# Attention group 15 on stacked split products, x_lo ahead of the query scaling on POOL, and two weight splits behind the token mixer's split on ScalarE

## The reference, cut to what is computed

```python
# 1. gated linear attention (mLSTM), B=2, H=8, S=768, head_dim 40, step by step over t:
m_new = max(f + m, i);  f_stab = exp(f + m - m_new);  i_stab = exp(i - m_new)
C = f_stab * C + i_stab * outer(v, k);   n = f_stab * n + i_stab * k
y[t] = sigmoid(o_gate) * (C @ q) / max(|n @ q|, 1)
# 2. mixer block on x = y as (B, S, 320): over tokens (768 -> 256 -> 768), then channels (320 -> 1536 -> 320)
h = relu(xT @ w_tok1) @ w_tok2;  u = x + hT;  x = u + relu(u @ w_ch1) @ w_ch2
# 3. x + real(FFT over channels of FFT over tokens); layer norm; channel MLP (320 -> 1280 -> 320)
```

## Time and profile before

| | us |
|---|---|
| median of 3 runs | 372.11 (371.92 to 373.74) |
| the profiled execution | 373.46 |
| its span, first to last instruction | 371.60 |
| PE busy | 362.3 (98%) |
| DVE / ACT / POOL busy | 190.5 / 155.5 / 129.3 |

### The profile page before, as it was taken

One profiled execution on the slowest core, in us unless ns is written; L12 is line 12 of the kernel. 1 busy time (PEld: TensorE's weight loads), 2 busy tenths in 40 slices (PEclk: granted clock), 3 DMA queues, 4 the chain that ended last, 5 costly groups with the idle time before them and its releaser, 6 DMA issues.

```text
span 371.6 us, 6184 instructions
## 1 busy us (share of the span) xinstructions
PE 362.3 (98%) x2371; PEld 350.9 (94%) x2371; DVE 190.5 (51%) x403; ACT 155.5 (42%) x325; POOL 129.3 (35%) x128
## 2 busy tenths in 40 slices
PE   8999998999999999999999999999999999999996
PEld 3788897899999999999999999999999999999996
DVE  7878753655343442154951486447934475331321
ACT  4678797789673232011441144505305202320310
POOL 6348886988987100010045200734414000000000
PEclk9999999999999999999999999999999999999999
DMA  7978999661535000003032100614050101001000
GB/s 161 246 171 231 235 298 274 186 197 55 146 88 146 19 0 2 18 30 116 1 108 71 56 0 3 228 54 160 2 167 29 35 3 53 2 15 40 0 19 35
DMA packets 18752, 34.36 MB, mean 92 GB/s; under 512 B 2636, under 2 KB 7892, under 8 KB 18724
## 3 DMA queue, kind: packets, MB, share of 16 engines
q1 hardware_dynamic: 17652, 32.40, 30.7%
q0 software_dynamic: 352, 1.31, 1.3%
q10 hardware_dynamic: 720, 0.27, 0.4%
HBM read 29.35 MB, written 4.62 MB: 91 GB/s over the span
## 4 chain that ended last, share of the span: by engine, by line
PE 83%; ACT 4%; DMA 2%; DVE 1%; issue 1%; SPq 0%; ACTq 0%; DVEq 0%
PE ps L712 31%; PE ps L689 25%; PE ps L692 4%; PE ps L691 4%; PE ps L647 3%; PE ps L571 3%; PE ps L814 3%; PE ps L795 2%; PE ps L665 2%; DMA og<-in_o 2%; PE ps L556 2%; PE ps L625 1%; PE ps L581 1%; PE ps L544 1%; PE ps L527 1%
## 5 line engine op out<-in xcount | busy, mean ns | idle before, releaser
L1009 ACT ACTIVATE h_hi<-ps 128x384 fp32r<-128x384 f32 x88 | 43.2, 491 | 116.3 <-PE ps L692 116.2
L1259 DVE SCALAR_TENSOR_TENSOR h_lo<-ps,h_hi 128x384 fp32r<-128x384 f32 x88 | 48.8, 555 | 55.0 <-ACT h_hi L1009 53.7
L1265 DVE TENSOR_TENSOR xt<-ps,xt 128x320 f32<-128x320 f32 x24 | 11.8, 491 | 65.5 <-PE ps L712 65.5
L712 PE MATMUL ps<-ch_hi,h_hi 128*128 128x320 f32 x144 | 45.1, 313 | 0.0
L712 PE MATMUL ps<-ch_hi,h_lo 128*128 128x320 f32 x144 | 44.5, 309 | 0.0
L712 PE MATMUL ps<-ch_lo,h_hi 128*128 128x320 f32 x144 | 44.5, 309 | 0.0
L712 PE MATMUL ps<-m_hi,h_hi 128*128 128x320 f32 x120 | 37.4, 312 | 0.0
L712 PE MATMUL ps<-m_hi,h_lo 128*128 128x320 f32 x120 | 37.1, 309 | 0.0
L712 PE MATMUL ps<-m_lo,h_hi 128*128 128x320 f32 x120 | 37.0, 309 | 0.0
L689 PE MATMUL ps<-uT_hi,ch_hi 128*128 128x384 f32 x96 | 32.5, 338 | 0.3 <-DVE xt L1428 0.3
L689 PE MATMUL ps<-uT_lo,ch_hi 128*128 128x384 f32 x96 | 32.1, 335 | 0.0
(11 more groups left out here) (172 smaller groups left out, 888.4 us busy)
## 6 DMA issues: line engine op xcount, KB each, us to landing
ch_raw<-in_ch SPq DMA_DIRECT2D x11, 384.0 KB, 6.9
vk<-in_vk SPq DMA_DIRECT2D x12, 328.0 KB, 4.5
raw<-in_kq SPq DMA_DIRECT2D x16, 240.0 KB, 3.6
m_raw<-in_m SPq DMA_DIRECT2D x11, 320.0 KB, 4.5
kq<-in_kq SPq DMA_DIRECT2D x16, 192.0 KB, 5.0
og<-in_o SPq DMA_DIRECT2D x12, 160.0 KB, 4.9
x_scratch<-xt SPq DMA_DIRECT2D x12, 160.0 KB, 2.3
out<-xt SPq DMA_DIRECT2D x12, 160.0 KB
```

The costliest lines, as they stand in the source:

```text
L712: mm = pe.matmul(bank, h[hx][:, f, i * P:(i + 1) * P], w[wx][:, f], start=(f == 0 and hx == 0 and wx == 0), stop=(f == FCH[k] - 1 and hx = ...
L1009: act.activation(h[0][:, f], h_bank(k, f), ACT.Relu).then_inc(hhi_done, 1)
L1259: dve.scalar_tensor_tensor(out=h[1][:, f], in0=h_bank(k, f), scalar=0.0, in1=f32(h[0][:, f]), op0=ALU.max, op1=ALU.subtract).then_inc(hlo_ ...
L1265: dve.tensor_tensor(xt[:, tile], o_bank(n), xt[:, tile], ALU.add).then_inc(o_done, 1)
```

## The change

`STACKED` goes from 16 to 15, so products(15) take four stacked matmuls, and group 15 gets a load, a rounding and a subtraction of its own. The host lays out one more group of `kq3`. The buffers move, since chunk 7's `kq` is still in use by group 14: the odd `kq3` buffers now lie over `kq` of even chunks, the even `raw3` buffers over both. `load_qk` still runs up to chunk 7.

```diff
+SPLIT_BEHIND = (12, 13)
+STACK_FIRST = {13: (15,)}
-STACKED = 16
+STACKED = 15
...
-    raw3 = [[at(f"raw3_{x}_0", o + 2048 * x, [P, 4 * CH]),
+    raw3 = [[at(f"raw3_{x}_0", o + 4096 + 2048 * x, [P, 4 * CH]),
...
-    kq3 = [[at(f"kq3_{x}_{n}", o + (8192, 4096)[n] + 2048 * x, [P, 4 * CH], F32R) for n in range(2)]
+    kq3 = [[at(f"kq3_{x}_{n}", o + (8192, 0)[n] + 2048 * x, [P, 4 * CH], F32R) for n in range(2)]
...
                 if n < STACKED + 2:
-                    sp.wait_ge(qk_done, STACKED - 2)
+                    sp.wait_ge(qk_done, (NG // 2, STACKED)[n - STACKED])
...
-                if cc + 1 < STACKED // 2:
+                if cc + 1 <= STACKED // 2:
                     load_qk(cc + 1)
...
-                act.wait_ge(qk_done, max(n - 1, STACKED))
+                act.wait_ge(qk_done, n - 1)
...
-                    if m < N_CH2:
+                    if m < N_CH2 and m not in SPLIT_BEHIND:
                         split_hi(m)
...
             attend(13)
+            stack_hi(15)
             attend(14)
             mixed_hi(0)
+            for m in SPLIT_BEHIND:
+                split_hi(m)
             attend(15)
...
+                if g == 1 and cc == NC:
+                    result_lo(cc - 1)
+                for m in STACK_FIRST.get(n, ()):
+                    pool.wait_ge(xlo_done, cc)
+                    stack_lo(m)
                 if g == 1 and cc >= NC and c < NC - 1:
                     scale_q(cc + 1)
...
-                if g == 1 and cc >= NC:
+                if g == 1 and cc > NC:
                     result_lo(cc - 1)
```

## The result

| | before | after |
|---|---|---|
| median (us) | 371.94 (20 executions, 371.45 to 373.74) | 374.82 (20 executions, 372.5 to 377.99) |
| profiled execution, its own time | 373.46 | 375.56 |
| its span | 371.6 | 373.8 |
| mean granted clock | 1.000 | 0.991 |

The ratio is 1.0066 [1.0054, 1.0079], which is 2.5 us of loss [2.0, 2.9]. The forecast was +1.0 us, 373.1, with a range to 374.4: the sign was right and the size was not. The median lies above the range; 371.94 times the ratio is 374.4, just at its end. The wide spread is new too. The executions differ in their mean clock: five of the 20 have 0.998 or more, with a median of 372.8; nine have 0.995, with a median of 374.7; six have 0.991, with a median of 375.5. By these medians, the lower the mean clock, the longer the time.

A forecast was written before the change was run, and what follows sets the result against it. PE was taken to bound the kernel: −1.61 − 0.46 − 0.42 (old waits, shorter products) + 2.99 (new waits ahead of mix_back) + 0.5 (wait at products(16)) = +1.0 us, so 373.1; range 371.2 to 374.4.

The forecast's parts named there:

- The bound: PE, busy 362.3 of 371.6 us; a shift of its work at 76 us should reach the end whole.
- x_lo first: On POOL, x_lo ahead of qs, there at about 58.1: PE's 1.61 us wait goes, mix_tokens(0, 5) starts at 61.0.
- Loads of group 15: In SP's queue ahead of eAb and og: 2.0 us more (bounds 1.3 to 2.9); raw(15) at 60.2, og at 62.5.
- stack_hi(15) ahead of attend(14): On ACT, waits for raw(15): W(14) 4 us later, at 61.3, so in_chunk(14) starts at 65.0, not 63.8.
- Two splits behind hp: On ACT, two ch_hi moved behind hp take 1.5 us off the 4.59 us from gate to hp_hi.
- mix_back(0): On PE: starts at 66.7 against 66.22, +0.5, with about 3.0 us of waits between 62 and 66.7.
- stack_lo(15) on POOL: 2.7 us more on POOL makes stack_lo(16) late, at 76.1; products(16) on PE wait 0.5 us, start at 76.2, +1.0.
- my signs of being wrong: Wrong if raw(15) lands before 59, if products(16) have no wait, or if ACT waits for raw(17).
- Raw(17), rival (c): Raw(17), issued behind stack_lo(15), delays ACT and products(16): shift 2.1 to 5.9 us, 374.2 and more; chance 0.19 with slow queue.

The follow-up runs named there:

- e5: The kernel before, unchanged, profiled once more: 372.32 us, ratio 1.0002.
- e2: The kernel before with only the two changes of order (x_lo first, two splits behind hp_hi), no group 15: 371.64 us, ratio 0.9992.
- e4: The kernel before plus two unused 240 KB loads where the changed kernel issues raw(15): 374.88 us, ratio 1.0070.
- e6: The kernel before plus the two unused loads of e4 and eight unread matmuls on PE ahead of mix_tokens(0, 5): 374.88 us, ratio 1.0084.
- e3: The changed kernel with stack_hi(15) behind W(14) and the mask on ACT instead of ahead of them: 374.08 us, ratio 1.0052.
- e10: The changed kernel with eight unread matmuls in PE's wait ahead of in_chunk(14), run again beside e9 on one chip: 373.12 us, ratio 1.0034.
- e1: The changed kernel with eight unread matmuls put into PE's wait ahead of in_chunk(14): 373.97 us, ratio 1.0039.
- e9: The changed kernel, unchanged, run again beside e10 on one chip: 374.5 us, ratio 1.0080.
- e11: e2 plus six mask copies on ACT ahead of attend(14), making W(14) late without added loads: 374.49 us, ratio 1.0096.
- e12: e11 plus eight unread matmuls in PE's wait ahead of in_chunk(14): 373.18 us, ratio 1.0036.
- e7: The changed kernel with weight loads 9 and 10 issued a chunk later, behind raw(15), eAb and og: 371.87 us, ratio 0.9994.

## Why the prediction was wrong in size

By its own steps:

- **The bound.** Right. PE's row decides, and a shift at products(16) reaches the end: +2.58 us there (77.82 against 75.24), +2.2 in the span, so 0.4 was made up behind it.
- **x_lo first.** Right in mechanism: it runs at 57.4 (forecast 58.1) and PE's wait is gone. Wrong in worth: 1.61 us was one execution's value, e5 has 0.94. The smaller gain was always there to be had; the order alone (e2) shows 0.3 us, which can't be told from none.
- **Loads of group 15.** Right in place, a little large in size. I took 2.0 us in bounds of 1.3 to 2.9. Where ACT waited for og itself it came at 60.90 (e4), 61.29 (e6) and 61.33 (e3), against 59.70 and 59.73 without the loads (e5, e2): 1.2 to 1.6 us. (Against the 60.54 of the first trace it would be half of that or less.) Raw(15) was down by 58.8 to 59.6 in the runs of this form, not 60.2. The Trainium skill (DMA: Bandwidth & Descriptors, Specifications) gives about 358 GB/s for a core, from which the prediction estimated 1.4 us; these landings agree with it, although the stretch of raw loads alone shows 247 GB/s.
- **stack_hi(15) ahead of attend(14).** Right: W(14) at 60.7 (61.3), in_chunk(14) at 64.45 (65.0), with PE idle for 2.00 us ahead of it.
- **Two splits behind hp.** Right: hp at 64.94, 0.19 us earlier than the earlier trace rows, in spite of a gate 1.3 us later.
- **mix_back(0).** 67.04 against 66.7 in the profiled execution, but for another reason: 0.9 us of it is in_chunk(14) and products(15) at half clock. At full clock it starts at 65.6 to 65.9 (e10, e1).
- **stack_lo(15) on POOL.** Right where the clock holds: products(16) wait 0.26 and 0.30 us for POOL (e1, e10; forecast 0.5). With the clock down PE comes later than POOL, and the wait is swallowed. No wait of products(16) was one of my signs of being wrong, and the profile after shows none: there POOL's row did not set the time, the clock did.
- **Raw(17), rival (c).** Didn't happen, ACT doesn't wait. Its figure, 374.0 and more, was met by another mechanism, so that is no support for it.
- **The term that was missing.** The sum moved instructions about and kept their durations. Its +1.0 us (+0.3 to +1.9) is close to what the filled kernels measure, 1.5 and 1.3 us, and to the executions of the changed kernel at full clock, 0.9. In part that is luck: the gain of x_lo was set 0.7 us too high and the delay of og 0.4 to 0.8 too high, and in the sum the two errors offset each other. On top comes the clock: 1.0 us between the changed kernel and e1, 1.7 between e9 and e10, 2.2 between e11 and e12. I had written down about 3 us of PE waits between 62 and 66.7, and read the 1.00 of the granted clock in the stretches of before, but never asked whether the clock would outlast the longer wait: the step that failed is the term for TensorE's clock, put at nothing without a reason. Nothing in the trace of before could have given the price, since there a wait of 1.61 us passed without a fall; a rival with this mechanism, and an upper end above 374.4, belonged in the range.

Two things stay open. The loads alone cost 2.6 us in the median even at full clock (e6) where the profiled executions and their traces show 1.6; there the fall of the clock had no price in the median. And the wait of 2.00 us sometimes leaves the clock alone, and sometimes costs 3.4 and sometimes over 6.5 us at half clock, which no row here explains.

No version beats the kernel before by more than can be measured: the order alone gives 371.64, with the pieces moved 371.74, the whole change with the pieces moved 371.87.

## What to carry to other kernels

In this queue, busy nearly throughout, two loads put ahead of others made those behind them land 1.2 to 1.6 us later. So where a load is added to a full queue, ask which of those loads a bounding engine waits for, and move the load that nobody waits for (e7) rather than the engines' order. When a change gathers TensorE's short waits into a longer one, give the clock a term in the sum of its own; a few matmuls that nobody reads, put into the wait, tell whether it is the clock or the work. A wait further on can swallow a part of the clock's price (e4 and e6). And take the waits of the profile from more than one execution before an edit's worth is set at them: here they were 2.07 us in one and 1.42 in the next.

## What was not expected of the hardware

After an idle time of 2.00 us, with TensorE busy on both sides of it, the granted clock stood at 0.50 for over 6.5 us in one execution and for 3.4 us in another, and in others not at all. The median paid 1.0 to 2.2 us for it in three pairs of kernels (the changed kernel and e1, e9 and e10, e11 and e12) and nothing in a fourth (e4 and e6). Eight matmuls of 128x512 put into the wait kept the clock at full in all 28 executions of e1, e10 and e12.
